# The first load of a one-core kernel as two transfers of the same columns: partitions 0 to 15, then partitions 16 to 127

## The chip, the cores and the metric

The kernel runs on one core of one Trainium2 chip. The metric is the device time of one execution in microseconds (us), the median of several runs. A core has five engines with instruction streams of their own: TensorE (PE, whose weight loads are listed as PEld), VectorE (DVE), ScalarE (ACT), GpSimd (POOL) and SyncE (SP). SP computes nothing here; it issues transfers, which 16 DMA engines carry out.

## The reference

Linear attention for 8 batches of 8 heads over 576 positions of 64 dimensions, an RMS normalization, and a soft mixture of 8 experts over all 4608 tokens of 512 dimensions:

```python
kv = np.einsum('bhsd,bhse->bhde', k, v)
out = np.einsum('bhsd,bhde->bhse', q, kv)
x = out / sqrt(mean(out * out, -1) + 1e-6) * g_norm     # then (4608, 512)
logits = x @ phi                                        # 32 slots, 4 for each expert
d = softmax(logits, axis=0); slot_input = d.T @ x
slot_out[e] = maximum(slot_input[e] @ w1[e], 0) @ w2[e]
result = softmax(logits, axis=1) @ slot_out
```

All of it is float32. Inputs and output together are about 71 MB, almost half of it the weights w1 and w2.

## The kernel before

**Stages.** Per batch b the products k by v are summed over positions (class Kv: products, borders, slots), and give block matrices bd that q is multiplied with, 36 tiles of 128 tokens in all. Each tile is squared, normalized and reduced to logits. Groups of six tiles keep a running maximum and a running sum of d.T @ x. After the last tile come the experts (expert_h and expert_y), then the mix and the stores.

**Memory.** Nearly everything that is loaded lies in one tensor in the core's memory, arena, of 128 partitions by 144 + 40,960 floats. Its first 144 columns (HEAD) hold phi and g_norm. Behind them are rows of kv, q and weights, each of which is loaded over what is no longer needed. The input in_first holds those 144 columns and the first half of the k and v of batch 0, 2,304 columns: 2,448 floats for each of 128 partitions. Its transfer is line 344. The other half of batch 0 is kv0 (in_kv0, in the views under in_kv), loaded by line 345; then come kv1, q0 and kv2 (lines 346 to 348), and all later loads follow at places of the program that line 351 and the calls of load_w give.

**Order and waits.** The function writes no waits. Its nc is an Order (line 120), which records each call as an Op in program order and works out what it must wait for: settle keeps the waits that are not implied by earlier ones, and emit issues the instructions, a wait on the last needed semaphore being part of the instruction itself. Each transfer has a semaphore of its own, dma_ and the number of the Op. Which calls touch the same bytes is found from Memory (line 77): it keeps, for each column and each group of 32 partitions, the last writer and the last readers. cells (line 88) turns a region into groups with

```python
return slice(first // 32, last // 32 + 1), np.unique(at // (self.bank or 1))
```

and add (lines 162 to 165) makes a call that writes a region wait for the writer that stands there, if it is on another engine or is a transfer:

```python
for w in np.unique(m.writer[rows, cols]):
    if w >= 0 and (self.ops[w].engine != engine or self.ops[w].dma):
        deps.add(int(w))
```

An engine runs its instructions in order, so an instruction that waits holds all behind it on that engine.

**The start.** Before the first data are there, PE runs products on a tensor of zeros and on one of ones (lines 712 and 713: five of the one, two of the other form, whose results nobody reads; a float32 product stands twice in the trace). DVE builds gphi from phi and g_norm (line 381). Then the loop of line 715 takes batch 0 in two halves: g = 0 reads what in_first brought, g = 1 what kv0 brought. After each half two or no products on ones follow (EARLY). All stores but three small ones on POOL are issued by SP too, the last three of them as rows of 128 partitions.

Of the kernel before, what the change touches and what calls it, by code (L numbers as in the profile page):

```python
# [63 lines left out]
HEAD = 144  # L64
# [224 lines left out]
def soft_moe_linear_attention(nc, first_in, kv0_in, kv_in, q0_in, kv2_in, kv4_in, kv5_in, t3_in, w_in, out):  # L289
# [5 lines left out]
    arena = const.tile([P, HEAD + ARENA], F32, name="arena")  # L295
# [9 lines left out]
    def load_row(at, src):  # L305
        nc.sync.dma_start(place(at, src.shape[-1]), src)
# [34 lines left out]
        return parts[k][:, at : at + 256]  # L341


    nc.sync.dma_start(arena[:, : HEAD + 2304], first_in)
    load_row(KV_AT[0] + 9, kv0_in)
    load_row(KV_AT[1], kv_in[0])
    load_row(Q_AT[0] + 8, q0_in)
# [678 lines left out]
def build_program():  # L1026
    import concourse.bacc as bacc

    nc = bacc.Bacc("TRN2", target_bir_lowering=False, num_devices=1, dynamic_dma_scratch_size=SCRATCH)
    shapes = {  # L1030
        "first": (P, HEAD + 2304), "kv0": (P, 2304 + 2048), "kv": (2, P, TOK), "q0": (P, 2560),
        "kv2": (P, TOK + 2048),
        "kv4": (P, 2560 + TOK), "kv5": (P, 2 * TOK), "t3": (P, 3 * TOK),
        "w": (1, 2 * NE * P * UNIT),
    }
    args = [nc.dram_tensor(f"in_{n}_dram", s, F32, kind="ExternalInput").ap() for n, s in shapes.items()]
    args.append(nc.dram_tensor("out_0_dram", (1, 4 * NCH * P * 4 * CT * NS), F32, kind="ExternalOutput").ap())
    order = Order(nc)
    soft_moe_linear_attention(order, *args)
    order.emit()  # L1040
    return nc
# [62 lines left out]
```

How the kernel before makes its waits and increments, by code:

```python
    def emit(self):  # L204
        nc = self.nc
        counters = {e: nc.alloc_semaphore(f"done_{e}") for e in ENGINES[:4]}
        sems = list(counters.values())
        counts = dict.fromkeys(counters, 0)
        for op in self.ops:
            method, args, kwargs = op.call
            engine = getattr(nc, op.engine)
            *before, last = sorted(op.waits, key=lambda w: w.i) or [None]
            for w in before:
                engine.wait_ge(w.sem, w.value)
            inst = getattr(engine, method)(*args, **kwargs)
            if last is not None:
                inst.wait_op(last.sem, last.value, "sem-ge")
            if op.dma:
                op.sem, op.value = nc.alloc_semaphore(f"dma_{op.i}"), 16
                sems.append(op.sem)
                inst.then_inc(op.sem, 16)
            elif op.signals:
                counts[op.engine] += 1
                op.sem, op.value = counters[op.engine], counts[op.engine]
                inst.then_inc(op.sem, 1)
        *stores, last = [op.sem for op in self.ops if op.dma and not op.signals]
        numbers = sorted(s.num for s in sems)
        assert numbers == list(range(numbers[0], numbers[-1] + 1)) and numbers[-1] == last.num
        for sem in stores:
            nc.sync.wait_ge(sem, 16)
        nc.sync.sem_clear(range(numbers[0], last.num))
        nc.sync.wait_ge(last, 16)
        nc.sync.sem_clear(range(last.num, last.num + 1))
```

## Time and profile before

| | us |
|---|---|
| time, median of 3 runs | 171.65 |
| the three runs | 171.57 to 171.8 |
| the profiled execution, its own time | 171.73 |
| its span, first to last instruction | 170.4 |
| PE busy | 151.0 |
| ACT busy | 88.5 |
| DVE busy | 86.9 |
| POOL busy | 59.6 |
| mean of what the DMA engines moved | 421 GB/s |

The profile is of one execution. Its page gives each engine's busy time, the span in 40 slices with the busy share in tenths, and the chain of work that ended last. Other views of the trace give the instructions in order of time, the issues of transfers with the time to their landing, and busy times by stretch.

### The profile page before, as it was taken

The numbers are of one execution on the slowest core, as the hardware profiler recorded it, in microseconds if no ns is written. First come the engines' busy times: TensorE is split into PE (matmuls) and PEld (weight loads), VectorE is DVE, ScalarE is ACT, GpSimd is POOL, SyncE is SP. The second block draws the span as 40 slices with busy tenths as digits, with TensorE's granted clock in tenths as the row PEclk, the third lists the DMA queues.
The fourth block names the chain that finished last, engine by engine and source line by source line (L and its number), as shares of the span: only waits on it lengthen the run. The fifth ranks groups of instructions, "written<-read, shape, count | busy, mean of one in ns | idle before, by whom it ended". The sixth has DMA issues, their size and how long they took to land.

```text
span 170.4 us, 4234 instructions
## 1 busy us (share of the span) xinstructions
PE 151.0 (89%) x1834; PEld 104.0 (61%) x1834; DVE 86.9 (51%) x185; ACT 88.5 (52%) x230; POOL 59.6 (35%) x73
## 2 busy tenths in 40 slices
PE   7998998999999899999899989989999989989200
PEld 3457987979688888796696664345566533454000
DVE  1111437743677265763936798724888036319300
ACT  3015778786965887768849864202234044418300
POOL 7000247757356755366482589300000004000000
PEclk9999999999999999999999999999999999999855
DMA  5999999999999999999999999999999999999996
GB/s 193 440 435 417 478 413 409 457 430 478 419 415 439 432 441 413 419 400 460 400 458 408 448 408 423 431 458 396 431 427 431 452 435 396 427 415 439 415 447 288
DMA packets 3933, 71.65 MB, mean 421 GB/s; under 512 B 742, under 2 KB 742, under 8 KB 874
## 3 DMA queue, kind: packets, MB, share of 16 engines
q1 hardware_dynamic: 3562, 71.18, 97.8%
q8 instruction: 14, 0.23, 0.5%
q0 software_dynamic: 352, 0.20, 0.4%
q14 instruction: 5, 0.04, 0.1%
HBM read 61.94 MB, written 9.44 MB: 419 GB/s over the span
## 4 chain that ended last, share of the span: by engine, by line
PE 54%; DMA 16%; ACT 15%; DVE 6%; issue 1%; SPq 0%
PE psum L215 54%; DMA arena<-in_w_dram 10%; DMA arena<-in_kv_dram 6%; ACT bd L215 4%; ACT sq L215 4%; ACT xall L215 2%; DVE ms L215 2%; DVE logits L215 1%; ACT part L215 1%; ACT arena L215 1%; ACT r L215 1%; ACT d L215 1%; DVE part L215 1%; DVE acc L215 1%; DVE r L215 0%
## 5 line engine op out<-in xcount | busy, mean ns | idle before, releaser
L215 PE MATMUL psum<-bd,arena 128*128 128x192 f32 (+1 forms) x320 | 56.6, 336 | 2.4 <-ACT bd L215 1.2
L215 PEld LDWEIGHTS psum<-bd,arena 128*128 128x128 f32 (+1 forms) x320 | 45.5, 179 | 9.7 <-ACT xall L215 3.5
L215 DVE TENSOR_REDUCE ms<-sq 128x16 f32<-128x1024 f32 (+1 forms) x19 | 22.1, 1162 | 28.6 <-ACT sq L215 28.5
L215 POOL TENSOR_TENSOR part<-part,r 128x512 f32<-128x512 f32 x17 | 17.8, 1047 | 48.9 <-DVE r L215 48.9
L215 POOL TENSOR_TENSOR xall<-xall,r 128x512 f32<-128x512 f32 x34 | 34.7, 1042 | 0.0
L215 ACT ACTIVATE sq<-psum 128x512 f32<-128x512 f32 x36 | 21.5, 596 | 9.0 <-PE psum L215 8.9
L215 PEld LDWEIGHTS psum<-arena 128*64 128x64 f32 (+1 forms) x640 | 18.8, 137 | 6.6 <-issue 3.0
L215 PE MATMUL psum<-arena 128*64 128x64 f32 (+1 forms) x640 | 21.4, 226 | 0.3 <-DMA arena<-in_kv_dram 0.3
L215 ACT COPY xall<-psum 128x512 f32<-128x512 f32 x34 | 20.7, 608 | 0.0
L215 ACT COPY part<-psum 128x256 f32<-128x256 f32 (+1 forms) x38 | 13.7, 359 | 9.2 <-DVE part L215 8.0
L215 DVE TENSOR_REDUCE logits<-part 128x64 f32<-128x512 f32 (+1 forms) x18 | 17.8, 991 | 0.0
L215 PE MATMUL psum<-arena,xall 128*32 128x256 f32 x256 | 15.0, 380 | 0.4 <-DMA arena<-in_w_dram 0.4
L215 DVE COPY arena<-psum 128x768 f32<-128x768 f32 (+1 forms) x12 | 10.5, 889 | 6.8 <-PE psum L215 6.8
L215 ACT COPY arena<-psum 128x768 f32<-128x768 f32 (+1 forms) x14 | 10.2, 754 | 7.1 <-PE psum L215 7.1
L215 PE MATMUL psum<-logits,part 32*128 32x384 f32 x96 | 12.7, 527 | 0.6 <-ACT arena L215 0.4
L215 POOL DMA_DIRECT2D out_dram<-arena x2 | 1.2, 589 | 33.8 <-DVE arena L215 33.8
L215 PE MATMUL psum<-arena,sq 128*32 128x256 f32 x224 | 12.7, 379 | 0.2 <-DVE sq L215 0.2
L215 PEld LDWEIGHTS psum<-arena,xall 128*32 128x32 f32 x256 | 8.1, 110 | 6.9 <-issue 1.4
L215 PE MATMUL psum<-xall,d 128*32 128x258 f32 x144 | 10.8, 390 | 1.0 <-ACT d L215 1.0
L215 ACT COPY bd<-psum 64x128 f32<-64x128 f32 (+1 forms) x32 | 9.8, 308 | 2.4 <-PE psum L215 2.2
L215 PEld LDWEIGHTS psum<-arena,sq 128*32 128x32 f32 x224 | 7.2, 110 | 5.1 <-DVE sq L215 0.5
L215 ACT COPY kvT<-psum 128x256 f32<-128x256 f32 (+1 forms) x9 | 3.1, 348 | 12.6 <-PE psum L215 12.5
(80 smaller groups left out, 129.7 us busy)
## 6 DMA issues: line engine op xcount, KB each, us to landing
arena<-in_w_dram SPq DMA_DIRECT2D x4, 4096.0 KB, 23.8
arena<-in_w_dram SPq DMA_DIRECT2D x4, 2048.0 KB, 20.5
arena<-in_t_dram SPq DMA_DIRECT2D x1, 6912.0 KB, 35.6
arena<-in_w_dram SPq DMA_DIRECT2D x2, 3072.0 KB, 22.9
arena<-in_kv_dram SPq DMA_DIRECT2D x2, 2304.0 KB, 19.0
arena<-in_kv_dram SPq DMA_DIRECT2D x1, 4608.0 KB, 40.3
arena<-in_kv_dram SPq DMA_DIRECT2D x1, 3584.0 KB, 29.9
arena<-in_kv_dram SPq DMA_DIRECT2D x1, 3328.0 KB, 26.0
```

Source lines behind the costliest of these rows:

```text
L215: inst = getattr(engine, method)(*args, **kwargs)
```

## The change

The call for in_first is written twice, for its first 16 partitions and for the other 112, with the same columns:

```diff
-    nc.sync.dma_start(arena[:, : HEAD + 2304], first_in)
+    nc.sync.dma_start(arena[:16, : HEAD + 2304], first_in[:16])
+    nc.sync.dma_start(arena[16:, : HEAD + 2304], first_in[16:])
     load_row(KV_AT[0] + 9, kv0_in)
     load_row(KV_AT[1], kv_in[0])
     load_row(Q_AT[0] + 8, q0_in)
```

The built program's rows of SP, at its start, before (partitions by floats, and in brackets the semaphores waited for):

```order
L215 DMA arena<-in_first_dram 128x2448 [waits barrier_Pool_Activation_PE_DVE_SP_release]
L215 DMA arena<-in_kv_dram 128x4352
L215 DMA arena<-in_kv_dram 128x4608
L215 DMA arena<-in_q_dram 128x2560
L215 DMA arena<-in_kv_dram 128x6656
```

And after:

```order
L215 DMA arena<-in_first_dram 16x2448 [waits barrier_Pool_Activation_PE_DVE_SP_release]
L215 DMA arena<-in_first_dram 112x2448 [waits dma_0]
L215 DMA arena<-in_kv_dram 128x4352
L215 DMA arena<-in_kv_dram 128x4608
L215 DMA arena<-in_q_dram 128x2560
L215 DMA arena<-in_kv_dram 128x6656
```

The second of the two transfers stands ahead of the four other loads, and waits for dma_0, the semaphore of the first.

On PE, where the products of batch 0 wait for their data, the difference of the two programs (- before, + after; the numbers count all recorded calls):

```order
 L215 MATMUL psum<-ones 128x512 [waits done_gpsimd]
 L215 MATMUL psum<-ones 128x512
-L215 MATMUL psum<-arena 64x64 [waits dma_0]
+L215 MATMUL psum<-arena 64x64 [waits dma_1]
 L215 MATMUL psum<-arena 64x64 x19
 L215 MATMUL psum<-zeros 128x512
```

The first product on loaded data waits for the second of the two transfers; nothing changes its place. DVE's first instruction on gphi does the same. Every later transfer's number is higher by one, and no instruction of PE, DVE, ACT or POOL stands elsewhere than before.

## Rows read from the trace of the kernel before

**Rows 1.** The page: span, engines, slices with DMA and GB/s, SP's queue.

```profile
span 170.4 us, 4234 instructions
PE 151.0 (89%) x1834; PEld 104.0 (61%) x1834; DVE 86.9 (51%) x185; ACT 88.5 (52%) x230; POOL 59.6 (35%) x73
DMA  5999999999999999999999999999999999999996
GB/s 193 440 435 417 478 413 409 457 430 478 419 415 439 432 441 413 419 400 460 400 458 408 448 408 423 431 458 396 431 427 431 452 435 396 427 415 439 415 447 288
DMA packets 3933, 71.65 MB, mean 421 GB/s; under 512 B 742, under 2 KB 742, under 8 KB 874
q1 hardware_dynamic: 3562, 71.18, 97.8%
```

**Rows 2.** The chain that ended last: start us, us, what.

```profile
0.74 0.38 SPq L215
1.18 9.99 DMA arena<-in_kv_dram
11.17 0.04 issue
11.21 1.47 PE psum L215 x40
...
117.08 17.48 DMA arena<-in_w_dram
134.56 0.14 issue
134.70 1.97 PE psum L215 x32
```

**Rows 3.** The end: SP's timeline, issues with us to landing, busy times by stretch.

```profile
155.28 0.34 SPq L215 DMA_DIRECT2D out_dram<-arena  x1
159.42 0.33 SPq L215 DMA_DIRECT2D out_dram<-arena  x1
...
out_dram<-arena SPq DMA_DIRECT2D x1, 1536.0 KB, 7.8
out_dram<-arena SPq DMA_DIRECT2D x1, 3072.0 KB, 10.9
...
core 0: us, PE busy (x) PEld busy (x) DVE busy (x) ACT busy (x) POOL busy (x), PEclk, DMA share, GB/s
160.00:168.00 8.00, 0.00 (x0) 0.00 (x0) 0.00 (x0) 0.00 (x0) 0.00 (x0) 0.53 1.04 449
168.00:169.00 1.00, 0.00 (x0) 0.00 (x0) 0.00 (x0) 0.00 (x0) 0.00 (x0) 0.50 0.80 344
169.00:170.00 1.00, 0.00 (x0) 0.00 (x0) 0.00 (x0) 0.00 (x0) 0.00 (x0) 0.50 0.06 25
```

**Rows 4.** SP's timeline of the first 3 us: start, us, issue (in_kv: kv0 and kv1, then kv2).

```profile
0.74 0.38 SPq L215 DMA_DIRECT2D arena<-in_first_dram  x1
1.18 0.89 SPq L215 DMA_DIRECT2D arena<-in_kv_dram  x2
2.12 0.64 SPq L215 DMA_DIRECT2D arena<-in_q_dram  x1
2.80 0.44 SPq L215 DMA_DIRECT2D arena<-in_kv_dram  x1
```

**Rows 5.** Busy times by stretch of the first 5 us, columns as in rows 3.

```profile
1.00:1.75 0.75, 0.69 (x2) 0.28 (x3) 0.41 (x3) 0.75 (x1) 0.48 (x3) 1.00 0.00 0
1.75:2.00 0.25, 0.25 (x2) 0.11 (x1) 0.16 (x1) 0.25 (x1) 0.03 (x1) 1.00 2.48 392
2.00:2.25 0.25, 0.25 (x2) 0.04 (x1) 0.00 (x0) 0.02 (x1) 0.25 (x2) 1.00 0.00 0
2.25:2.50 0.25, 0.25 (x2) 0.15 (x1) 0.00 (x0) 0.00 (x0) 0.25 (x2) 1.00 0.85 235
...
4.00:5.00 1.00, 1.00 (x3) 0.46 (x2) 0.00 (x0) 0.00 (x0) 0.10 (x1) 1.00 1.01 431
```

**Rows 6.** Issues of the first 3 us: KB, us from issue to landing.

```profile
arena<-in_first_dram SPq DMA_DIRECT2D x1, 1224.0 KB, 5.3
```

**Rows 7.** PE's timeline of the first 14 us: start, us, what.

```profile
3.17 3.62 PE L215 MATMUL psum<-ones 128*128 128x512 f32 x4
6.71 1.52 PE L215 MATMUL psum<-arena 128*64 128x64 f32 x40
...
9.01 1.88 PE L215 MATMUL psum<-ones 128*128 128x512 f32 x4
```

**Rows 8.** A load that reuses a freed buffer, at 101.66: issue and us to landing.

```profile
101.66 0.33 SPq L215 DMA_DIRECT2D arena<-in_w_dram  x1
...
arena<-in_w_dram SPq DMA_DIRECT2D x1, 3072.0 KB, 18.2
```

## The prediction

> **What bounds the kernel now.** I read the page's slices first, since they tell which resource is full for how long. The DMA line shows 9 in every slice but the first, which has 5, and the last, with 6; the mean is 421 GB/s and SP's hardware queue q1 alone holds 97.8% of the engines' span [rows 1]. So the transfers are one unbroken stream from the first packets to about 169 us, and a stream without holes ends later by as much as it starts later. TensorE (PE) is busy too, 89% [rows 1], so I then read the chain of waits to see whether PE could set the end alone. It begins with SP's first issue at 0.74, goes over the transfer of kv0 that lands at 11.17, runs along PE, and at 117.08 enters a weight transfer that lands at 134.56 and releases PE at 134.70 [rows 2]. Both ends of that chain are transfers: PE starts on one and is held up by another. PE cannot run ahead of a late stream.
>
> The end says the same. SP issues the last store at 159.42 and it lands 10.9 later, at 170.3; the store before it was issued at 155.28 and landed 7.8 later, at 163.1. The engines move 449 GB/s through 160 to 168 with DMA share 1.04, and only in 168 to 170 do they run dry [rows 3]. The last store therefore waits in a full queue, not for its data.
>
> **What the change does.** The words say two transfers; the program's rows say more. SP's second row now carries a wait for dma_0, which is the first row's own transfer. The cause is in the recording layer: it books arena in groups of 32 partitions, partitions 0 to 15 and 16 to 127 meet in group 0, and a write over cells that a transfer wrote waits for that transfer (the rule in add for the writer of out). No engine reads anything between the two. So SP stands still until 16 rows have landed, and behind it in SP's order stand the loads of kv0, kv1, q0 and kv2, whose issues now lie at 1.18 to 3.24 [rows 4], so that nothing else can fill the 16 engines. PE and DVE, which waited for the one first transfer, wait for the second one.
>
> **The start before, by its terms.** SP's issue starts at 0.74 [rows 4]. No packet begins in the stretch up to 1.75; in 1.75 to 2.00 the engines take up 392 GB/s x 0.25 us = 98 kB, which is 10 rows of 9,792 bytes (2,448 floats); in 2.00 to 2.25 none; in 2.25 to 2.50 235 x 0.25 = 59 kB, 6 rows. That view books a packet where it begins. Ten and six are 16, one for each engine [rows 5]. Hence:
> - issue to first packet: 1.75 - 0.74 = 1.01 us, and six engines begin 0.5 later;
> - a first row takes long, with nothing in flight ahead of it: the ten 2.48 x 16 x 0.25 / 10 = 0.99 us, the six 0.85 x 16 x 0.25 / 6 = 0.57 us [rows 5];
> - a later row: at 431 GB/s an engine moves 26.9 GB/s, so 9,792 bytes take 0.364 us [rows 5];
> - end of data to landing: the latest engine begins by 2.50 and is done by 2.50 + 0.57 + 7 x 0.364 = 5.62; the transfer lands 5.3 after 0.74, at 6.04 [rows 6]. So 0.42 us, at the least.
>
> **The start after.** The 16 rows are the first row of each engine, and I give them the times that those rows have now: the last ends at 2.50 + 0.57 = 3.07, and lands at 3.07 + 0.42 = 3.49. SP resumes 0.04 later, as PE does after kv0's landing [rows 2]: 3.53. The second transfer's packets begin 1.01 after that: ten engines at 4.54, six at 5.04. Each engine has 7 rows left, as before, since 112 is 7 times 16; the engines have been idle, so the first of these rows takes 0.57 instead of 0.364 (0.21 more). I take 0.57 and not 0.99 because the slow ten may hold something paid once in a program. Before, the second rows began at 1.75 + 0.99 = 2.74 on ten engines and 2.25 + 0.57 = 2.82 on six. The shift is 4.54 + 0.21 - 2.74 = 2.01 us on ten, 5.04 + 0.21 - 2.82 = 2.43 on six, and (10 x 2.01 + 6 x 2.43) / 16 = 2.17 on the mean. Everything behind follows without a gap, because the four next loads are issued within about 2 us, as now, and the second transfer gives 2.5 us of data.
>
> The bounds. Low: all 16 first rows begin together at 1.75 and take 0.57, land at 2.32 + 0.42 = 2.74, SP resumes at 2.78, packets begin on all engines at 3.79 with rows of 0.364; against a mean of 2.77 before, the shift is 1.0. High: the second issue takes 0.64, as q0's does, and not 0.38 [rows 4], 0.26 more, and ten engines pay 0.99 again, 0.42 x 10 / 16 = 0.26 more: 2.7.
>
> For the restart, the Trainium skill (DMA: Bandwidth & Descriptors, Specifications) gives about 0.6 us to the first byte for transfers issued from SP. The rows above have 1.01 from the start of the issue instead; by the skill's page the sum would be 0.4 lower, 1.8. I go by the rows.
>
> **What compute does with it.** PE takes the first rows at 6.71 although they had landed at 6.04, because its warm-up products on ones run until 3.17 + 3.62 = 6.79 [rows 7]; so 0.7 of the shift is hidden there, and PE then idles from 6.79 to about 8.2. This gains nothing: PE's next stop is kv0, landing at 11.17, PE taking it up at 11.21 [rows 2], and that landing moves by the full 2.2. From there PE runs as before, 2.2 later. Would the stream run dry where SP waits for PE to free a buffer? The load issued at 101.66 (3,072 KB) lands 18.2 us later [rows 8]; at the mean of 421 GB/s its own data take 7.5 us, so it stands about 10.7 us in the queue. Some microseconds of lateness of PE reach no such load. At the end, the last store could send packets at 159.42 + 1.01 = 160.43, while the store ahead occupies the engines to about 163.1 - 0.42 = 162.7: 2.3 us of margin.
>
> **The sum.** The profiled execution took 171.73, of which 170.4 is the span; the 1.3 around it is untouched. 171.73 + 2.17 = 173.9. The profiled run stands 0.08 over the median of 171.65, so the median to expect is 173.8.
>
> **The rivals.**
> - *A cheap restart*: short first rows, no stagger, no second fill of an empty pipe. This is the low bound: 171.65 + 1.0 = 172.7. For it: the six later engines took 0.57. Against it: the 1.01 and the 0.42 are paid in any case, and nothing suggests that 16 rows leave faster than the first 16 of 128. Up to 1.5 of shift I count as this.
> - *PE falls behind further.* The warm-up products of the same form took 3.62 / 4 = 0.905 us at the start and 1.88 / 4 = 0.47 at 9.01 [rows 7], which I read as the lower and the higher level of PE's clock (1.2 and 2.4 GHz), though the granted clock stands at 1.00 in the windows from 1 to 5 us [rows 5]. With PE idle for 1.4 us the clock may fall back. If the 4.2 us of work from 6.71 to 10.89 doubled from 8.2 on, PE would be free at 8.2 + 8.4 = 16.6 instead of finding kv0 at 13.4: 3.2 late, against the 2.3 of margin at the end: 0.9 more, 174.7, and beyond if it lasts. It decides only when lateness exceeds 2.3 us. Against it: the 1.4 us of idling follows 5.7 us of unbroken work.
> - *No wait in effect, not slower*: what the change's words say. The two transfers follow each other, the ten and six engines all begin at 1.75, and the mean engine gains 6 x 0.5 / 16 = 0.19: 171.5; with the added issue delaying kv0's descriptors and nothing gained, 171.65. It decides if the first transfer has landed when SP comes to its second row, at about 1.2. Its first packet begins only after 1.75, so this needs the wait not to be there. The Trainium skill (DMA: Bandwidth & Descriptors, Rules for kernel authors) says that two transfers to disjoint partition halves only serialize on the same 16 engines; by that alone the time would be this rival's 171.65, and the rows decide against it because of the wait.
> - *The stream catches up, not slower*: to make up 2.17 us in 170 the mean rate must rise by 1.3%, from 421 to 427 GB/s. Slices vary between 396 and 478 [rows 1]. Against it: the engines show no idle time in between that a later start could use.
>
> **How the numbers follow.** The forecast, a shift of 1.5 to 2.7: 0.72. Cheap restart: 0.14. PE behind: 0.09. Not slower: 0.05, for both ways together. The range leaves out the last of these and the far end of PE's: 172.7 (shift 1.0) to 174.7. A measurement here can tell about 0.2%, 0.34 us, from no change. Forecast, cheap restart and PE all lie over that: slower 0.95. Of the rest, 171.65 and 171.5 both lie within it; I leave 0.03 for same and 0.02 for faster.
>
> **What will show it.** In SP's timeline the second issue starts at about 3.5 and not at 1.2, with a wait on the transfer of in_first_dram of about 2.4 us. A few packets begin at 1.75 to 2.5, then none until about 4.5. The first landing that PE waits for comes at about 8.2, kv0's at 13.3, the last load's and the last store's about 2.2 later too, with the DMA slices at 9 in between. It is wrong if SP issues the second transfer before 2.7, if kv0 lands 2.2 later but the last store does not, or if the clock drops between 7 and 15.

## The result, and the profile after

The changed kernel takes 175.43 us (median of 4 runs, 175.33 to 176.25) against 171.73 for the kernel before. The ratio is 1.0228, with a 95% interval of 1.0212 to 1.0243: slower by 3.7 us. The forecast was slower, by 2.1 us to 173.8, with a range up to 174.7. The direction held; the size did not, and the time lies outside the range.

The page of the changed kernel, the lines that answer to [rows 1] (span, slices with DMA share and GB/s, SP's queue):

```profile
span 174.1 us, 4235 instructions
DMA  1999999999999999999999999999999999999996
GB/s 36 271 368 442 409 469 414 418 445 421 496 402 462 421 423 445 388 459 405 444 414 433 444 410 423 422 442 429 416 425 437 459 420 403 429 406 439 428 446 299
q1 hardware_dynamic: 3578, 71.18, 96.6%
```

The first slice (4.35 us) is nearly empty, which is the wait. The second slice is the surprise. Its DMA digit is 9, so the engines were busy, but it moved 271 GB/s where the kernel before had 440. From the fourth slice on both kernels move alike.

The end answers to [rows 3]. The busy times by stretch, columns as there, SP's timeline, and the last two stores with KB and us from issue to landing:

```profile
164.00:172.00 8.00, 0.00 (x0) 0.00 (x0) 0.00 (x0) 0.00 (x0) 0.00 (x0) 0.54 1.04 449
172.00:173.00 1.00, 0.00 (x0) 0.00 (x0) 0.00 (x0) 0.00 (x0) 0.00 (x0) 0.50 0.69 295
...
159.51 4.48 SPq L215 DMA_DIRECT2D out_dram<-arena  x2
...
out_dram<-arena SPq DMA_DIRECT2D x1, 3072.0 KB, 10.4
out_dram<-arena SPq DMA_DIRECT2D x1, 1536.0 KB, 7.3
```

It is the same picture 3.7 us later, with the same 449 GB/s: the last store still waits in a full queue.

The start answers to [rows 4] and [rows 6]. SP's timeline, SP's wait (total, times, longest), and the issues with KB and us to landing:

```profile
0.74 3.36 SPq L215 DMA_DIRECT2D arena<-in_first_dram  x2
4.14 0.91 SPq L215 DMA_DIRECT2D arena<-in_kv_dram  x2
...
SPq L215 <- DMA arena<-in_first_dram: 2.6, 1, 2.6
...
arena<-in_kv_dram SPq DMA_DIRECT2D x1, 2176.0 KB, 11.7
arena<-in_first_dram SPq DMA_DIRECT2D x1, 1071.0 KB, 6.9
arena<-in_first_dram SPq DMA_DIRECT2D x1, 153.0 KB, 3.0
```

SP waits 2.6 us for the first 16 rows, as the order of instructions said it would, and issues kv0 at 4.14 instead of 1.18. The 153 KB land 3.0 us after their issue at 0.74. The 1,071 KB land 6.9 us after theirs at 3.77, at 10.7, where the forecast had 8.2. Why that transfer is so slow stands in the stretches that answer to [rows 5] (columns as there):

```profile
1.75:2.00 0.25, 0.25 (x2) 0.11 (x1) 0.16 (x1) 0.25 (x1) 0.03 (x1) 1.00 1.84 470
2.00:2.25 0.25, 0.25 (x2) 0.04 (x1) 0.00 (x0) 0.02 (x1) 0.25 (x2) 1.00 0.30 118
3.00:3.50 0.50, 0.50 (x2) 0.41 (x2) 0.00 (x0) 0.00 (x0) 0.50 (x2) 1.00 0.00 0
4.50:5.00 0.50, 0.50 (x3) 0.19 (x1) 0.00 (x0) 0.00 (x0) 0.00 (x0) 1.00 1.74 274
5.00:6.00 1.00, 0.57 (x2) 0.00 (x0) 0.00 (x0) 0.00 (x0) 0.00 (x0) 1.00 0.42 147
6.00:7.00 1.00, 0.00 (x0) 0.00 (x0) 0.00 (x0) 0.00 (x0) 0.00 (x0) 1.00 1.11 411
7.00:8.00 1.00, 0.00 (x0) 0.00 (x0) 0.00 (x0) 0.00 (x0) 0.00 (x0) 0.81 1.16 274
8.00:9.00 1.00, 0.00 (x0) 0.00 (x0) 0.00 (x0) 0.00 (x0) 0.00 (x0) 0.50 1.20 299
9.00:10.00 1.00, 0.00 (x0) 0.00 (x0) 0.00 (x0) 0.00 (x0) 0.00 (x0) 0.50 0.76 246
```

The last two columns, DMA share and GB/s, together give the time of one row. An engine that moves rate / 16 while it is busy for the share needs 9,792 x 16 x share / rate for a row. In 6 to 7 that is 9,792 x 16 x 1.11 / 411e3 = 0.42 us, near the 0.364 of before; in 7 to 8 it is 0.66. The engines are not short of work. They are slow. The first rows after the pause are slow too: 14 rows begin in 4.50 to 5.00 (274 x 0.5 / 9.792), and each takes 9,792 x 16 x 1.74 / 274e3 = 0.99 us. The same sum is used below for every run.

### The profile page after: what moved, and what is told of

It is laid out like the page before. It is cut to its first block, busy times and chain, and to the rows that moved or that the text cites. A ratio compares the mean times of both kernels' runs of the same rounds, so it can differ in the third digit from the quotient of the medians.

```text
span 174.1 us, 4235 instructions
## 1 busy us (share of the span) xinstructions
PE 150.8 (87%) x1834; PEld 105.2 (60%) x1834; DVE 86.9 (50%) x185; ACT 88.6 (51%) x230; POOL 59.7 (34%) x73
## 4 chain that ended last, share of the span: by engine, by line
PE 66%; ACT 15%; DVE 6%; DMA 6%; issue 1%
PE psum L215 66%; DMA arena<-in_first_dram 6%; ACT bd L215 4%; ACT sq L215 4%; ACT xall L215 2%; DVE ms L215 2%; DVE logits L215 1%; ACT part L215 1%; ACT arena L215 1%; ACT r L215 1%; ACT d L215 1%; DVE part L215 1%; DVE acc L215 1%; DVE r L215 0%; DVE d L215 0%
## 5 line engine op out<-in xcount | busy, mean ns | idle before, releaser
L215 PE MATMUL psum<-arena 128*64 128x64 f32 (+1 forms) x640 | 22.2, 232 | 5.2 <-DMA arena<-in_first_dram 5.2
L215 PEld LDWEIGHTS psum<-arena 128*64 128x64 f32 (+1 forms) x640 | 19.7, 142 | 10.5 <-DMA arena<-in_first_dram 6.0
```

Source lines behind the costliest of these rows:

```text
L215: inst = getattr(engine, method)(*args, **kwargs)
```

## What was held against what

Two accounts were open after this. **Theory A**: the loss has two parts, SP's wait with its empty engines, and a slow transfer of 112 partitions, because, so the guess, 7 rows for each engine make engines write through the same ports of the core's memory. **Theory B**: the wait explains it all, and the slow rows are what a restart looks like. Further theories stand with the runs that test them.

## Undo the wait alone, and undo the split alone

Taking the wait away without a race needs a finer bookkeeping, so that the two transfers no longer share a group:

```diff
-        return slice(first // 32, last // 32 + 1), np.unique(at // (self.bank or 1))
+        return slice(first // 16, last // 16 + 1), np.unique(at // (self.bank or 1))
```

The arrays of writers and readers have 8 groups then, and the second transfer waits for nothing.

> The changed kernel with the bookkeeping in groups of 16 partitions in place of 32, so that the second transfer (partitions 16 to 127) no longer waits for the first; everything computed is the same. Theory A (two causes: SP's wait costs the 2.2 us of empty engines, and the transfer of 112 partitions itself runs slowly, its later rows 0.65 us instead of 0.37, because 7 rows for each engine make engines meet on the same write ports): the pause goes, the slow rows stay, so 172.7 to 173.5, with the landing that PE waits for at 7 to 8 us. Theory B (all of the loss comes from the wait; the slow rows are an after-effect of the restart): 171.4 to 171.8, landing at about 6.0.

Measured: 173.43 us, ratio 1.0089 (1.0066 to 1.0113), 2.0 below the changed kernel and 1.7 above the kernel before. The issues, and a stretch in which the 112 partitions are under way:

```profile
arena<-in_first_dram SPq DMA_DIRECT2D x1, 1071.0 KB, 7.1
arena<-in_first_dram SPq DMA_DIRECT2D x1, 153.0 KB, 3.4
...
5.00:6.00 1.00, 0.72 (x2) 0.00 (x0) 0.00 (x0) 0.00 (x0) 0.00 (x0) 1.00 1.03 264
```

There is no pause any more, and the rows still take 0.61 us. PE took the data up at 8.36, a little past the 7 to 8 expected for the landing. So the split without the wait costs 1.7 us, and the wait on top of it 2.0. The opposite run keeps the wait and gives up the split:

```diff
     nc.sync.dma_start(arena[:16, : HEAD + 2304], first_in[:16])
-    nc.sync.dma_start(arena[16:, : HEAD + 2304], first_in[16:])
+    nc.sync.dma_start(arena[:, : HEAD + 2304], first_in)
```

> The first 16 partitions are loaded as in the changed kernel, SP waits for them, and then all 128 partitions are loaded in one transfer (the 16 a second time, 153 KB more); everything computed is the same. Theory A (the 112-partition split is what makes rows slow after the restart): the second transfer starts at about 4.7 as in the changed kernel, all its rows after the first take 0.37, it lands at about 9.0 (5.2 after its issue), and the whole is 2.9 to 3.1 over before: 174.6 to 174.8, faster than the changed kernel although it moves more. Theory B (the slow rows come from the restart): rows of 0.65 again, landing at 10.7 or later, whole 175.6 to 176.2.

Measured: 174.85 us, ratio 1.0181 (1.0166 to 1.0196), 0.05 over the 174.6 to 174.8 of theory A, and 0.6 faster than the changed kernel although it loads 153 KB more. The issues and three stretches:

```profile
arena<-in_first_dram SPq DMA_DIRECT2D x1, 1224.0 KB, 5.4
arena<-in_first_dram SPq DMA_DIRECT2D x1, 153.0 KB, 3.1
...
4.50:5.00 0.50, 0.50 (x2) 0.13 (x1) 0.00 (x0) 0.00 (x0) 0.00 (x0) 1.00 0.95 137
6.00:7.00 1.00, 0.26 (x1) 0.00 (x0) 0.00 (x0) 0.00 (x0) 0.00 (x0) 1.00 1.03 431
7.00:8.00 1.00, 0.00 (x0) 0.00 (x0) 0.00 (x0) 0.00 (x0) 0.00 (x0) 1.00 1.04 441
```

After the same pause, the first rows are slow again (1.09 us for the seven that begin in 4.50 to 5.00), but the later ones take 0.37 us, and 128 partitions land 5.4 us after their issue, as before (5.3, [rows 6]). 112 partitions took 6.9. Theory B falls: a restart alone makes no slow rows after the first.

This run also prices the wait ahead of a whole load. It is 174.85 - 171.72 = 3.1 us over the kernel before, timed beside it, and one row more for each engine is 0.36 of that by [rows 5], so the wait costs about 2.8 there, and the split on top of it 3.7 - 2.8 = 0.9. Taken apart in the other order, it was 1.7 for the split and 2.0 for the wait. The two costs are not independent, and how the 3.7 divides depends on which is undone first.

## Other splits, and another source

If the partitions that meet are the cause, other splits should be slow too, each in its own measure. Partitions 0 to 31 and 32 to 127 share no group of the bookkeeping, so there is no wait:

```diff
-    nc.sync.dma_start(arena[:, : HEAD + 2304], first_in)
+    nc.sync.dma_start(arena[:32, : HEAD + 2304], first_in[:32])
+    nc.sync.dma_start(arena[32:, : HEAD + 2304], first_in[32:])
```

> The first load as partitions 0 to 31 and 32 to 127, 2 and 6 rows for each engine; the bookkeeping groups are not shared, so SP waits for nothing; everything computed is the same. Theory A (a transfer whose rows per engine are not the 8 of a whole 128-partition load makes engines meet on write ports): between the run of 16 and 112 without a wait (173.4) and the two halves (174.5), say 172.8 to 174.2, with rows of 0.5 to 0.75 us. Theory B (something peculiar to 16 or to 112 partitions): 171.5 to 172.0, rows of 0.37.

Measured: 173.44 us, ratio 1.0103 (1.0087 to 1.0118), as theory A had it. Halves, with 64 in place of 32:

> The first load in two halves, partitions 0 to 63 and 64 to 127, 4 rows for each engine in each; the bookkeeping groups are not shared, so SP waits for nothing; everything computed is the same. Theory A (engines that write partitions of one port share its rate): each half reaches half of the ports, so rows take about 0.73 instead of 0.37 for much of 8 rows, and the first landing that PE waits for comes 1.5 to 3 us later than 6.0; whole 173 to 174.6. Theory B (only the wait costs): 171.5 to 171.9.

Measured: 174.48 us, ratio 1.0191 (1.0134 to 1.0248; one of the four runs took 176.59), 2.8 over before with no wait at all. PE took the data up at 9.21, 3.2 after 6.0, a little past the 1.5 to 3 expected. A stretch of each, first of the 32 and 96, with rows of partitions 32 to 127 under way, then of the halves, with rows of 64 to 127:

```profile
5.00:6.00 1.00, 1.00 (x3) 0.21 (x1) 0.00 (x0) 0.00 (x0) 0.00 (x0) 1.00 0.94 235
```

```profile
5.00:7.00 2.00, 1.43 (x3) 0.21 (x1) 0.28 (x1) 0.00 (x0) 0.00 (x0) 1.00 0.96 211
```

Rows take 0.63 and 0.71 us. The halves come close to twice the 0.364 of a whole load, at about half its rate.

The slow rows could also come from the other end, from rows of the source that meet in HBM. So the source rows were put 10,240 bytes apart, in the run without a wait:

```diff
-        "first": (P, HEAD + 2304), "kv0": (P, 2304 + 2048), "kv": (2, P, TOK), "q0": (P, 2560),
+        "first": (P, HEAD + 2304 + 112), "kv0": (P, 2304 + 2048), "kv": (2, P, TOK), "q0": (P, 2560),
```

> The run of 16 and 112 partitions without a wait, with the source rows in HBM 10,240 bytes apart instead of 9,792; the destination and everything computed are the same. Theory A (the slow rows come from the destination, the partitions that engines write at one time): the same slow rows, whole 172.9 to 173.7. Theory C (they come from the source, rows of neighbouring engines meeting in HBM at this distance): rows and time change, towards 171.5 to 172.3 or well over 174.

Measured: 173.03 us, ratio 1.0080 (1.0065 to 1.0095), inside theory A's 172.9 to 173.7. In 5 to 6 us the share is 1.03 at 284 GB/s, 0.57 us a row. It stays slow; that pitch is not the cause. Other arrangements of the source were not tried.

The sharpest test takes 64 partitions again, but other ones. The Trainium skill (SBUF — State Buffer, Door 1: The DMA port swizzle) gives 16 ports for transfers, with a partition and the one 32 further on the same port within each half of 64. By that, 0 to 63 reach 8 ports and 32 to 95 reach all 16.

```diff
-    nc.sync.dma_start(arena[:, : HEAD + 2304], first_in)
+    for lo, hi in ((32, 96), (0, 32), (96, 128)):
+        nc.sync.dma_start(arena[lo:hi, : HEAD + 2304], first_in[lo:hi])
```

> The first load in three transfers without waits: partitions 32 to 95, then 0 to 31, then 96 to 127, that is 4, 2 and 2 rows for each engine; everything computed is the same. If write ports are shared as the Trainium skill says (SBUF: State Buffer, Door 1: 16 ports, a partition and the one 32 further on the same port within each half of 64), 64 partitions from 32 to 95 reach all ports, one for each engine, while 0 to 63 reach half of them. Theory A (shared ports, a matter of which partitions): the first transfer's rows take 0.37 after the first, and it lands 3.3 to 4.0 us after its issue, against 5.5 for partitions 0 to 63; the two of 32 partitions are slow (0.7), whole 172.8 to 173.8. Theory F (a transfer of 64 partitions is slow as such): 5.5 again, whole 174.4 or more.

Measured: 173.41 us, ratio 1.0094 (1.0072 to 1.0116), inside theory A's 172.8 to 173.8. The issues, a stretch with the 64 middle partitions under way, and one with the two groups of 32:

```profile
arena<-in_first_dram SPq DMA_DIRECT2D x1, 612.0 KB, 5.1
arena<-in_first_dram SPq DMA_DIRECT2D x2, 306.0 KB, 5.6
...
3.40:4.60 1.20, 1.20 (x2) 0.44 (x2) 0.00 (x0) 0.00 (x0) 0.70 (x3) 1.00 0.93 367
5.00:6.50 1.50, 1.20 (x3) 0.21 (x1) 0.00 (x0) 0.00 (x0) 0.00 (x0) 1.00 1.12 257
```

For comparison, the run of two halves while partitions 0 to 63 were under way:

```profile
3.40:4.60 1.20, 1.20 (x2) 0.44 (x2) 0.00 (x0) 0.00 (x0) 0.71 (x3) 1.00 1.19 245
```

Rows of the 64 middle partitions take 0.40 us where those of partitions 0 to 63 took 0.76, and the groups of 32 that follow take 0.68. (About a third of the rows in 3.40 to 4.60 are already of the next group; in 3.50 to 4.00, when not all of the 64 had begun yet, the share is 1.02 at 392 GB/s, 0.41 a row.) Theory F falls: not the number 64 is slow but which 64. In every run here row i of the source goes to partition i, so this run moved source and destination together. The pitch run speaks against the source; a run that parts the two was not made. One expectation failed. The first transfer landed 5.1 us after its issue, not 3.3 to 4.0; its rows were taken up quickly, and its last completion came late. That writes of the next transfers to the same ports delayed it is likely, but only argued.

## The late landing of the 16 rows

The 16 rows of the changed kernel landed about 1.1 us after their data were taken up: the last begins by 2.25, takes 0.30 x 16 x 0.25 / 3 = 0.40, and SP is released at 0.74 + 3.0. If it comes from the ports that 16 neighbouring partitions share, spreading the 16 should help. This is the run with 16 and then all 128, with the 16 taken from every eighth partition:

```diff
-    nc.sync.dma_start(arena[:16, : HEAD + 2304], first_in[:16])
+    nc.sync.dma_start(arena[::8, : HEAD + 2304], first_in[::8])
```

> As the run with 16 partitions and then all 128, but the 16 are every eighth partition (0, 8, ... 120) instead of 0 to 15; SP waits for them in the same way; everything computed is the same. Theory A (16 neighbouring partitions share few write ports, so that the small transfer lands about 1.15 us after its data were taken up instead of 0.4): spread over twice as many ports, the small transfer lands 2.3 to 2.6 us after its issue instead of 3.0, and the whole is 0.4 to 0.7 us below the run with partitions 0 to 15. Theory B (the small transfer's late landing is the fixed price of a lone transfer): 3.0 again and the same time.

Measured: 174.73 us (174.54 to 175.03), which overlaps the 174.71 to 174.91 of the run with partitions 0 to 15; in time this decides nothing. Its stretches and the landing, and then the stretches of the run with partitions 0 to 15:

```profile
2.00:2.25 0.25, 0.25 (x2) 0.04 (x1) 0.00 (x0) 0.02 (x1) 0.25 (x2) 1.00 1.12 313
2.25:2.50 0.25, 0.25 (x2) 0.15 (x1) 0.00 (x0) 0.00 (x0) 0.25 (x2) 1.00 0.84 235
2.50:2.75 0.25, 0.25 (x3) 0.01 (x1) 0.00 (x0) 0.00 (x0) 0.25 (x1) 1.00 0.19 78
...
arena<-in_first_dram SPq DMA_DIRECT2D x1, 153.0 KB, 2.9
```

```profile
1.75:2.00 0.25, 0.25 (x2) 0.11 (x1) 0.16 (x1) 0.25 (x1) 0.03 (x1) 1.00 1.95 548
2.00:2.25 0.25, 0.25 (x2) 0.04 (x1) 0.00 (x0) 0.02 (x1) 0.25 (x2) 1.00 0.11 39
```

The spread rows begin 0.25 to 0.5 us later, which takes most of the gain away. But their last ends by 2.75 + 0.38 = 3.13 and they land at 3.64, 0.5 after it; the neighbouring ones end by 2.25 + 0.44 = 2.69 and land at 3.84, 1.15 after it. So the tail of the landing shortened as theory A says, in one profile of each run. The landing expected 2.3 to 2.6 us after the issue was not reached (2.9), nor was the whole 0.4 to 0.7 us faster, and that ports are the reason is only argued.

## PE's clock

The clock did fall in the changed kernel: the stretches above grant 0.81 in 7 to 8 us and 0.50, the lower level of 1.2 GHz, from 8 on, after PE had stood idle since 5.6. PE's timeline, which answers to [rows 7]:

```profile
3.17 2.40 PE L215 MATMUL psum<-ones 128*128 128x512 f32 x4
10.74 2.40 PE L215 MATMUL psum<-arena 128*64 128x64 f32 x40 [5.18 <-DMA arena<-in_first_dram]
```

The same 40 products took 1.52 before. (The four warm-up products took 3.62 before, and the granted clock is 1.00 in the windows of both kernels there; why they differ was not followed up.) To see what this costs at the end, PE was given warm-up products to bridge the wait:

```diff
-    fill_wide(ps.tile([P, 512], F32, tag="m", name="fill"), 2)
+    fill_wide(ps.tile([P, 512], F32, tag="m", name="fill"), 7)
```

> The changed kernel with seven products on ones ahead of the first data instead of two, so that PE works until about 10.3 us, just before the data come at 10.7, and its clock has no reason to fall between 7.6 and 14.4; everything computed is the same. Theory A (the stream of transfers sets the end; in the changed kernel the last store is issued 163.7 and could send at 164.7, while the one ahead lands only at 166.8): 175.2 to 175.6, as the changed kernel, though PE is at the higher clock level from 7 us on. Theory D (the fallen clock is part of the 3.7 us): 173.9 to 174.9.

Measured: 175.46 us, ratio 1.0224 (1.0207 to 1.0241), against 175.43 of the changed kernel. A stretch and PE's timeline:

```profile
9.00:10.00 1.00, 0.83 (x2) 0.00 (x1) 0.00 (x0) 0.00 (x0) 0.00 (x0) 1.00 0.77 316
...
10.83 1.43 PE L215 MATMUL psum<-arena 128*64 128x64 f32 x40 [0.99 <-DMA arena<-in_first_dram]
```

The clock stays at 1.00, the products take 1.43 (1.52 before), and the time is the same. Theory D falls. As far as these runs can tell, the clock is no part of the 3.7 us.

## A split by columns

Last, a split that gives every engine its 8 rows in both transfers: the 144 columns of phi and g_norm, then the 2,304 of kv.

```diff
-    nc.sync.dma_start(arena[:, : HEAD + 2304], first_in)
+    nc.sync.dma_start(arena[:, :HEAD], first_in[:, :HEAD])
+    nc.sync.dma_start(arena[:, HEAD : HEAD + 2304], first_in[:, HEAD:])
```

> The first load split by columns instead of partitions: the 144 columns of phi and g_norm for all 128 partitions (576 bytes a row), then the 2,304 columns of kv for all 128; both have 8 rows for each engine, and the bookkeeping finds no overlap, so SP waits for nothing; everything computed is the same. Theory A (a split costs only by the partitions that it hands to each engine, or by a wait): 171.4 to 172.1, the small rows adding at most 0.4 us, rows of kv at 0.35. Theory E (any second issue at the start costs a microsecond or more of the stream): 172.7 or more.

Measured: 172.12 us, ratio 1.0026 (1.0015 to 1.0037): 0.5 over before, a hair over the top of theory A's range and far from theory E. DVE's gphi did start earlier by this, at 2.80 instead of 6.12, and the time shows no gain from it. No version tried beats the kernel before.

## Why the prediction was wrong, step by step

- **The stream without holes** held. The DMA digits of the changed kernel are 9 from the second slice on, and the last store is 3.7 us late with the same 449 GB/s behind it.
- **The wait** came as forecast, 2.6 us of SP's waiting against 2.4, but its price was too low. The forecast's whole shift of 2.17 stood for the wait ahead of rows at the old pace, and the run that is just that, with all 128 partitions behind the wait, gives about 2.8 (2.5 to 3.0 by its interval), at the high bound of 2.7. That undoing the wait of the changed kernel gains 2.0, close to 2.17, is a coincidence, since the slow rows stay in both.
- **The landing of the 16 rows** was off by two errors that partly cancelled. The rows began closer together than the first 16 of 128 had (12 in 1.75 to 2.00, by 470 x 0.25 / 9.792, against 10) and took 0.61 instead of 0.99, so they were done by about 2.65, not 3.07. Their landing took 1.1 more, not 0.42. SP resumed at 3.77, where the forecast had 3.53: 0.2 more.
- **The step that failed** is "Each engine has 7 rows left, as before, since 112 is 7 times 16", with 0.57 us for the first and 0.364 for each other. The count was right and the durations were not. The 0.364 was of a transfer of 128 partitions, and I carried it over to one of 112 without a bound of its own. In 5 to 8 us the engines take up 832 KB, 85 rows, at (0.42 + 1.11 + 1.16) x 16 / 85 = 0.51 us each, so six of them cost 6 x 0.14 = 0.9 more. The choice of 0.57 over 0.99 for the first row was wrong too: it took 0.99, 0.4 more. By these terms the shift is 2.2 + 0.2 + 0.4 + 0.9 = 3.7 us, an estimate from the stretches. The 0.9 is also what the split costs on top of the wait, by the runs. The 112 partitions landed 6.9 us after their issue, at 10.7 instead of 8.2.
- **The high bound** of 2.7 held a slower issue and a slower first row on ten engines. Nothing in it stood for the later rows or for a later landing of the 16, so the range stopped short.
- **The rival on PE** saw the clock fall, as it said it might, and a drop between 7 and 15 us was among the forecast's signs of being wrong. It came, but it was harmless, as the margin at the end said and the run with more warm-up products showed. The last store was issued at 163.7 (174.1 less the 10.4 of its row) and could send about 1.0 later, at 164.7; the store ahead of it landed only at 159.5 + 7.3 = 166.8.
- **The rival that names the Trainium skill** (DMA: Bandwidth & Descriptors, Rules for kernel authors), by which two transfers to disjoint partition halves serialize, and which the forecast read as no change in time, was set aside because of the wait. The halves show that this reading fails without a wait too: they cost 2.8 us.
- **kv0** landed at 4.14 + 11.7 = 15.8, 4.7 later than before, while the end is 3.7 later. A landing is that of the slowest engine; the stream as a whole was less late. Up to 40 us the kernel before moved 407 GB/s on the mean and the changed one 367, 1.6 MB less, which is 3.8 us at 421 GB/s. The two stretches, before and after:

```profile
0.00:40.00 40.00, 37.00 (x434) 27.95 (x434) 15.52 (x36) 22.47 (x61) 15.21 (x26) 1.00 0.96 407
0.00:40.00 40.00, 32.20 (x354) 24.55 (x355) 12.05 (x27) 18.16 (x48) 12.18 (x23) 0.91 0.91 367
```

## What to carry to other kernels

In a kernel whose transfers form one unbroken stream, look first at what a change does to that stream: a wait on the issuing engine ahead of all loads cost 2.0 to 2.8 us here, about the 2.6 that SP waited. Then give each new shape of transfer its own duration per row, and a bound for it, since the rate went here by which partitions a transfer covered; a load over all 128 partitions was the only one here that ran at full rate throughout, and 32 to 95 nearly did. A busy share of 9 does not mean full rate: read it with the GB/s beneath it.

## What the runs showed of the hardware

- Time per row of 9,792 bytes, after the first, by the partitions of one transfer: 0 to 127, 0.37 us; 32 to 95, 0.40; 16 to 127, 0.42 to 0.66; 32 to 127, 0.63; 0 to 31 and 96 to 127 behind 32 to 95, 0.68; the halves, 0.71 to 0.76.
- For the halves and for 32 to 95 this fits the ports of the Trainium skill (SBUF — State Buffer, Door 1: The DMA port swizzle) if consecutive rows go to one engine; the views don't show which engine wrote which partition, so that part is inferred. The fit is not complete. The same assumption would put two engines on each port in the whole load too, which ran at full rate, so its rows must be shared out in another way. For 16 to 127 it gives, as an estimate from the same table with the engines in step, 1.2 x 0.364 = 0.44 us a row, and the rows took 0.51 to 0.61 on the mean. What else slows the 112 partitions stays open.
- The Trainium skill (SBUF — State Buffer, "Can I just issue two DMAs to hit both halves?") says that only one transfer over all 128 partitions reaches all 16 ports. The 64 partitions from 32 to 95 moved 367 GB/s with the engines busy for 0.93 of the stretch, against 211 GB/s for a half, so in this case the measurement does not bear that out.
- A transfer of 16 neighbouring partitions landed 1.15 us after its last data had been taken up, and one of 16 spread partitions 0.5 us after.
- After a pause, first rows took about 1 us (0.99 for 14 engines in the changed kernel, 1.09 for seven in the run with all 128 partitions behind the wait), against 0.37 for later rows of a whole load.
